# Expert stage of a fused attention and mixture-of-experts kernel: rows gathered in quarters and turned by VectorE, rows stored times their gate

## The reference, cut to what matters

```
logits = x @ w_gate
expert_idx = argmax(logits, axis=1)
probs = exp(logits - max) / (sum(exp(logits - max)) + 1e-9)
gate_w = probs[arange(N), expert_idx]
for e in range(E):
    xe = x[mask]                       # rows whose expert is e
    h = maximum(xe @ w1[e], 0.0)       # 512 -> 1024
    ye = h @ w2[e]                     # 1024 -> 512
    out[mask] = gate_w[mask, None] * ye
```

## Time and profile before

| | us |
|---|---|
| median of 3 runs (lowest, highest) | 1504.67 (1502.96, 1509.15) |
| the profiled execution: its time | 1505.98 |
| the profiled execution: span from first to last instruction | 1504.3 |
| PE busy in the span | 1470.9 |
| mean granted TensorE clock | 0.994 |

### The profile page before, as it was taken

How to read it: one execution, slowest core, us unless ns; L and a number is a source line. 1 busy time by engine, 2 the same in 40 slices (tenths; PEclk the granted TensorE clock), 3 DMA queues, 4 the chain that set the end, 5 groups by cost and what they waited for, 6 DMA issues and landing times.

```text
span 1504.3 us, 29653 instructions
## 1 busy us (share of the span) xinstructions
PE 1470.9 (98%) x8062; PEld 1273.0 (85%) x8063; DVE 882.0 (59%) x1629; ACT 619.4 (41%) x1295; POOL 524.2 (35%) x653
## 2 busy tenths in 40 slices
PE   7999999999989999999999999999999999999996
PEld 6999999999978888888888888888788878888885
DVE  5688888888835474755647375536455545553332
ACT  5688788778812222121222212133344334442221
POOL 5676676676710021120202112021333333332321
PEclk9999999999999999999999999999999999999998
DMA  6353443444430202021120202144767666643441
GB/s 249 120 141 102 105 112 101 110 106 119 112 129 0 67 18 84 0 84 27 57 65 19 84 0 84 27 133 137 254 234 222 225 203 235 229 167 133 139 142 40
DMA packets 111242, 173.49 MB, mean 115 GB/s; under 512 B 52976, under 2 KB 72176, under 8 KB 106978
## 3 DMA queue, kind: packets, MB, share of 16 engines
q1 hardware_dynamic: 103618, 152.82, 32.9%
q0 software_dynamic: 7584, 20.17, 4.2%
HBM read 123.66 MB, written 50.34 MB: 116 GB/s over the span
## 4 chain that ended last, share of the span: by engine, by line
PE 60%; DMA 5%; issue 3%; SPq 2%; ACT 1%; DVE 1%; ACTq 0%; POOL 0%; DVEq 0%; POOLq 0%
PE bank L167 58%; DMA arena<-we 3%; SPq L824 1%; DMA arena<-h_scratch 1%; ACT arena L1252 1%; PE bank L1710 1%; DMA h_scratch<-arena 1%; SPq L1013 0%; SPq L1005 0%; SPq L990 0%; PE bank L1641 0%; DVE hturn L1484 0%; ACT big L810 0%; PE bank L1649 0%; PE bank L1660 0%
## 5 line engine op out<-in xcount | busy, mean ns | idle before, releaser
L167 PE MATMUL bank<-big,xs 128*128 (+1 forms) x2100 | 495.4, 395 | 15.5 <-DVE big L610 8.1
L167 PEld LDWEIGHTS bank<-big,xs 128*128 128x128 f32 x2100 | 394.1, 190 | 98.1 <-issue 15.9
L167 PE MATMUL bank<-xs,big 128*128 128x512 f32 x1728 | 397.2, 391 | 2.7 <-PEq L216 2.7
L167 PEld LDWEIGHTS bank<-xs,big 128*128 128x128 f32 x1728 | 324.6, 188 | 70.2 <-issue 3.0
L167 PE MATMUL bank<-big 128*128 128x512 f32 (+1 forms) x1632 | 324.6, 347 | 2.0 <-POOL big L306 1.4
L167 PEld LDWEIGHTS bank<-big 128*128 128x128 f32 (+1 forms) x1632 | 254.7, 164 | 36.2 <-POOL big L306 1.7
L1045 POOL TENSOR_TENSOR arena<-arena 128x512 f32<-128x512 f32 x32 | 39.9, 1257 | 438.9 <-DMA arena<-rec_scratch 438.9
L1427 DVE TENSOR_TENSOR arena<-arena,bank 128x512 f32<-128x512 f32 x72 | 49.5, 687 | 242.4 <-PE bank L167 242.4
L1352 DVE CUSTOM_DVE_ANT_0 arena<-arena 128x512 f32<-128x512 f32 x256 | 159.6, 689 | 15.9 <-ACT arena L1204 14.8
L1184 ACT COPY arena<-bank 128x512 f32<-128x512 f32 x72 | 42.4, 589 | 305.5 <-PE bank L167 301.1
L704 PE MATMUL bank<-arena 128*128 128x66 f32 (+1 forms) x1152 | 147.7, 269 | 0.0
(11 more groups left out here) (182 smaller groups left out, 1360.7 us busy)
## 6 DMA issues: line engine op xcount, KB each, us to landing
arena<-we SPq DMA_DIRECT2D x32, 1024.0 KB, 7.7
h_scratch<-arena SPq DMA_DIRECT2D x37, 512.0 KB
arena<-h_scratch SPq DMA_DIRECT2D x148, 128.0 KB
kqraw<-kq SPq DMA_DIRECT2D x32, 576.0 KB, 3.8
rows_scratch<-arena SPq DMA_DIRECT2D x36, 256.5 KB
xT_scratch<-arena SPq DMA_DIRECT2D x32, 288.0 KB
arena<-v SPq DMA_DIRECT2D x64, 128.0 KB, 2.4
arena<-xT_scratch SPq DMA_DIRECT2D x8, 1024.0 KB, 5.5
```

The costliest lines, as they stand in the source:

```text
L167: ins = nc.tensor.matmul(out, left[a], right[b], start=first and n == 0, stop=last and n == 2)
```

## The change

Before the experts, the gate is no longer the 513th number of a row: ACT multiplies the four tiles of `x2` by it in place (`gated`), and SP stores 512 numbers a row. The relus have no scale, and the copies of gates between engines are gone.

In the loop, TensorE's transposes of the gathered rows are gone. POOL gathers a tile in four indirect DMAs (`gather_quarters`): block b of columns of `xg` gets, on each quarter of 32 partitions, a quarter (128 numbers) of the rows whose place in the tile lies in quarter b. DVE turns the 32x32 blocks (`turn_rows`, STREAM_TRANSPOSE 128x512 into `xturn`), ACT and DVE split that into high and low part as before, now from SBUF. The lists of row numbers for the quarters (`idq`) are laid out once by 16 DMAs that SP issues between the stages. The columns of `w_out` and the rows of `w_gate` are permuted on the host to fit. Tiles 0 to 3 are still gathered whole and turned by TensorE.

SP's step is reordered: `store_rows(g)`, then `load_quarters(g)`, then `loads_of(g - 1)`.

```diff
@@ SP, stage2
-                    sp.wait_ge(x2_sb, BQ * i + q + 1)
-                    if q == 0:
-                        sp.wait_ge(gates_done, i + 1)
+                    sp.wait_ge(x2_gated, BQ * i + q + 1)
                     sp.dma_start(m["rows"][ds(i * BT + q * P, P), :], x2[:, q]).then_inc(rows_out, 16)
...
             def tile(g):
-                load_quarters(g - 1)
                 store_rows(g, hs)
+                load_quarters(g)
                 loads_of(g - 1)
...
             for c in range(CPE, CPE + 3):
                 load(c)
+            sp.wait_ge(idf_set, 1)
+            idq = m["idq"][:].bitcast(U32).rearrange("p (b n) -> p b n", b=NQ)
+            for a in range(NQ):
+                for b in range(NQ):
+                    sp.dma_start(idq[a * Q:(a + 1) * Q, b], m["idf"][b * Q:(b + 1) * Q, :]).then_inc(idq_in, 16)
             sp.wait_ge(w_lo, CPE)
             sp.wait_ge(idt_mm, 1)
             sp.wait_ge(tabs, 2)
+            store_rows(2, hq)
+            load_quarters(2)
             load(CPE + 3)
-            store_rows(2, hq)
@@ POOL
+            def gather_quarters(g):
+                row = table(m, pool, ROW, g, 0, E * TPE - 1)
+                if isinstance(g, int):
+                    pool.wait_ge(xtr_mm, g)
+                else:
+                    pool.wait_ge(x_turned, g)
+                pool.sem_inc(turn_taken, 1)
+                pool.tensor_tensor(m["idgq"][:], idq[:, :, ds(row, 1)].rearrange("p b n -> p (b n)"),
+                                   m["quarter"][:, 0:1].to_broadcast([P, NQ]), ALU.add).then_inc(idg_set, 1)
+                pool.wait_ge(idg_set, g + 1)
+                pool.sem_inc(turn_taken, 1)
+                for b in range(NQ):
+                    pool.indirect_dma_start(xg[:, b * P:(b + 1) * P], None,
+                                            m["rows"].rearrange("r (a n) -> (r a) n", a=NQ),
+                                            bass.IndirectOffsetOnAxis(m["idgq"][:, b:b + 1], 0)).then_inc(xq_in, 16)
...
             gather(FIRST)
-            gather(FIRST + 1)
+            pool.wait_ge(idq_in, 16 * NQ * NQ)
+            gather_quarters(FIRST + 1)
...
             def period(g):
-                gather(g + 2)
+                gather_quarters(g + 2)
                 scatter(g - 2)
@@ ACT
+            def gated(i):
+                act.wait_ge(gates_done, i + 1)
+                for q in range(BQ):
+                    act.mul(x2[:, q], x2[:, q], rq[:, 3, q:q + 1]).then_inc(x2_gated, 1)
+            def turned_rows_high(g):
+                act.wait_ge(x_turned, g + 1)
+                act.copy(m["xt"][:, 0], m["xturn"]).then_inc(xt_hi, 1)
...
                 relu_stored(g)
-                rows_high(g + 1, False)
-                next_gate(g + 1)
+                turned_rows_high(g + 1)
                 turned_h_high(g - 1)
@@ DVE
+            def turn_rows(g):
+                dve.wait_ge(xq_in, 16 * NQ * g - 16 * NQ * FIRST)
+                dve.wait_ge(h_mm, 2 * g)
+                dve.transpose(m["xturn"].rearrange("p (c b j) -> p c b j", c=DC, b=P // Q),
+                              xg.rearrange("p (b i c) -> p c b i", b=P // Q, c=DC)).then_inc(x_turned, 1)
...
             def tile(g):
-                rows_low(g + 1)
+                turn_rows(g + 1)
+                turned_rows_low(g + 1)
                 turn_h(g - 1)
@@ PE
                 for h in range(2):
                     first_product(g, h, *here)
-                x_transpose(g + 1)
                 second_product(g - 2, *before)
```

More of the change, by code:

```diff
@@ L52 @@
 BQ = BT // P
-XW = DM + 1
+XW = DM
 TPE = N // P
@@ L63 @@
 SLOTS = 4
+NQ = 4
 PARTS = ((0, 0), (0, 1), (1, 0))
@@ L109, in alloc @@
     over("hturn", [FF], xs_at + (DC * BT + DM) * 4)
+    over("xturn", [DM], xs_at + DC * BT * 4)
     over("filler", [XW], xs_at)
@@ L138, in alloc @@
     m["hq"] = arena[:, SLOTS * CW:SLOTS * CW + FF]
+    m["cden"] = m["idq"][:, 0:H * S // DK]
     m["gw"] = m["stage"][:, 0:GMAX * E]
+    m["gi"] = m["stage"][:, CW // 2:CW // 2 + GMAX * E]
+    m["idf"] = arena[:, SLOTS * CW + 2 * FF:SLOTS * CW + 2 * FF + E * TPE].bitcast(U32)
     at = CW - 2 * P
@@ L595, in _ @@
             dve.memset(v[0:D, :, MID + 1], 0.0).then_inc(masks_set, 1)
+            for a in range(NQ):
+                dve.memset(m["quarter"][a * (P // NQ):(a + 1) * (P // NQ), :], a)
             def w3_low(j):
@@ L846, in stage2 @@
         idg_set, ids_set, turn_taken = sem("s3_idg_set"), sem("s3_ids_set"), sem("s3_turn_taken")
-        gate_set, relu_done = sem("s3_gate_set"), [sem(f"s3_relu_done{h}") for h in range(2)]
-        h_turned, gate_saved = sem("s3_h_turned"), sem("s3_gate_saved")
+        relu_done = [sem(f"s3_relu_done{h}") for h in range(2)]
+        h_turned, x_turned = sem("s3_h_turned"), sem("s3_x_turned")
+        idf_set, idq_in, xq_in = sem("s3_idf_set"), sem("s3_idq_in"), sem("s3_xq_in")
+        x2_gated = sem("s2_x2_gated")
         h_stored, hq_in = sem("s3_h_stored"), sem("s3_hq_in")
@@ L1076, in ids_of, with gather @@
                 pool.tensor_copy(m["idg"][:], m["idall"][:, ds(row, 1)]).then_inc(idg_set, 1)
-            def gather_rows(g):
+            def gather(g):
+                pool.wait_ge(xtr_mm, g)
+                ids_of(g)
                 pool.wait_ge(idg_set, g + 1)
@@ L1140, in period @@
             def period(g):
-                gather(g + 2)
+                gather_quarters(g + 2)
                 scatter(g - 2)
             last = tiles(pool, period, 2)
-            keep_gate(last)
             scatter(last_of(pool, 3))
@@ L1186, in turn @@
                         high(i, j - 1)
+                    if j == 4 and has_before(i):
+                        gated(i - 1)
                 high(i, FC - 1)
@@ L1251, in relu_half @@
                     product = product.rearrange("p (a k i) -> p a k i", a=2, i=Q)
-                act.activation(out, product, ACT.Relu, scale=m["gate"][:, 0:1]).then_inc(relu_done[h], 1)
+                act.activation(out, product, ACT.Relu).then_inc(relu_done[h], 1)
                 if h == 1:
@@ L1708, in x_transpose @@
                 pe.wait_ge(gathered, 16 * g + 16)
+                by_chunk = xg.rearrange("p (n c) -> p c n", c=DC)
                 for c in range(DC):
-                    last = pe.transpose(xtr_ps[:, c * P:(c + 1) * P], xg[:, c * P:(c + 1) * P], m["ident"][:])
+                    last = pe.transpose(xtr_ps[:, c * P:(c + 1) * P], by_chunk[:, c], m["ident"][:])
                 last.then_inc(xtr_mm, 1)
```

72 lines of the change are left out of this document (27 added, 45 removed).

## The result

The changed kernel takes 1512.62 us (median of 7 runs, 1511.4 to 1513.94), the kernel before 1506.29 us in the same series (7 runs, 1502.96 to 1509.19). The ratio is 1.0041 with a 95% interval of 1.003 to 1.0053. That is 0.4% slower: measurable here, but under the 0.5% that the prediction set as its bound for "slower", and about half of the 0.9% forecast. The profiled execution of the changed kernel has a span of 1512.2 us against 1504.3 before, so 7.9 us are to be explained.

The account below looks back on a forecast made before the run. TensorE, busy in 98% of the span, bounds the kernel, and SP's new round the loaded steps: 3.3 + 14.4 - 4.7 = +13.0 us on a span of 1504.3, forecast 1517.5 us; range 1491 to 1531, the forecast's own 1512 to 1531.

Parts of the forecast that it names:

- the step that decides: SP's queue in loaded loop steps: waiting for its own store's landing makes a round of 12.3 us, against 11.0 for PE.
- 2.0 + 2.5: SP's round: four quarter loads 2.0 us, then table reads and address work 2.5 us, ahead of the weight load.
- 20 steps from tile 6 on, +14.4: Loop steps holding 20 of 24 weight loads: 245.6 us with SP's new round against 231.2 before.
- in between: Rival for SP's round in the loop: 11.6 us a round, total about the same, 1504 us; chance 0.20.
- 36 x 0.36: Four TensorE transposes removed in each of the loop's 36 steps, 0.36 us a step: 13.0 us saved.
- lie beside products of 5 us: nothing: Dense blocks: ACT's eight times four gate multiplications, 0.6 us each, cost nothing.
- The ninth delays the last stores of rows: End of the dense blocks: ACT's ninth set of gate multiplications makes the last row stores some 1.6 us later.
- Lists and tile 4: Between the stages: 16 list DMAs at 0.5 us each delay tile 4's first product by 7.2 us; +8.9 with the clock.
- the rival of POOL's round: Loop: gathers stuck behind weight loads make POOL's round the bound, 11.9 us, 1515 us, up to 1540; chance 0.12.
- What would show it: Trace signs: four-group L1710, SP waiting for store landings, PE waiting 1.3 us a step, 8 us gap before tile 4.
- the faster rival: SP's round fits at 11.2 us: -12.7 us, 1492 us; sign: SP waits for the turn, PE unbroken; chance 0.28.

Follow-up runs that it names:

- g_whole_rows: Of the change only rows stored times their gate, scaled one copy earlier; whole gathers, TensorE transposes, old SP order: 1502.11 us, 0.9981 to the kernel before.
- b_new_sp: The kernel before with only SP's step in the changed order (store, its own quarters, weight load): 1504.71 us, ratio 0.9995.
- g_old_sp: The changed kernel with the gate scaling one copy earlier and SP's step in the old order: 1494.69 us, 0.9937 to the kernel before.

## Why the prediction was right or wrong, point by point

**The total.** The forecast was +13.0 us of span, measured +7.9; 1512.62 us lies in the range and at the edge of the forecast's own range (1512 to 1531). The sign was right, but that is luck in good part: two errors of 10 and 14 us, of opposite signs, nearly cancelled, so the total proves little. (By its own sum the forecast is 1504.67 + 13.0 = 1517.7 us and not 1517.5, which changes nothing.)

**SP's reordering, "the step that decides".** Mechanism right for the first half of the loaded steps: SP waits for its store's landing instead of for relus, the next quarters go out 7.56 us behind the weight load (foreseen 7.6 + 0.2), and undoing the order gives 10 to 12 us. Size wrong: the term "2.0 + 2.5" between quarters and weight load measured 3.94 us, of which the quarter loads are 1.92, so the table reads and address work take 2.0 us. The 2.5 us had been read between a store and a weight load, another place in the queue. The round is 11.50 and not 12.3 us. The failed step of the sum is "20 steps from tile 6 on, +14.4": it is +0.3 (ledger). 19 x 0.8 = 15.2 us for the shorter round cover the whole difference of 14. The prediction had written that a tenth in the round is 1.9 us; in effect its rival "in between" (a round of 11.6) describes the loop that ran.

**Transposes.** 36 x 0.36 was too small: a step without them is 10.88 us, not 11.0, so each step had spent 11.36 - 10.88 = 0.48 us on them, 17 us in all. The time from a group's start to the next matmul (0.35) left out the rest: the 48 matmuls up to the next group take 1140.99 - 1129.99 = 11.00 us, and without groups 10.88. Over the last 12 steps 5.3 us came back, where 4.7 were foreseen for 13.

**The transition.** The step that failed outright is "lie beside products of 5 us: nothing" together with "The ninth delays the last stores of rows". All nine sets of multiplications delay stores, and the eighth puts the last-but-one block's stores among the id scatters. The loss is 9.8 us there, by the start of tile 0's transposes, before and after:

```profile
1008.54 0.60 PE L1710 MATMUL bank<-ident,arena 128*128 128x128 f32 x4
```

```profile
1018.29 0.64 PE L1738 MATMUL bank<-ident,arena 128*128 128x128 f32 x4
```

1.9 of these were there before the gap's cause, the rest is the gap and the slow clock behind it. Both experiments that change the order of the two transfers take 0.4 to 0.5% back. The prediction asked whether ACT had time for the work and not what goes out later because of it.

**Lists and tile 4.** Foreseen +7.2 us for tile 4's start; measured 1079.67 - 1062.40 - 9.8 = 7.5. That is close only because errors cancel again: an issue took 10.62 / 16 = 0.66 us and not 0.5, over the upper bound of 9 us for the sixteen, and the four gathers took 5.9 us from 1067.80 on, the first of them 2.16 beside VectorE's work; but the copies began 4.8 us sooner than foreseen (1052.57 against 1047.6 + 9.8), since the third weight load was out sooner. That in turn is because the last rows land 4.2 us behind their first store's issue, here and in g_whole_rows, where the rows of 513 numbers took 9.2 us (8.2 in b_new_sp); the prediction had taken the 9.2 over. At tile 6 the loss without the transition is 13.9 - 9.8 = 4.1, foreseen 3.3.

**VectorE's turn.** Taken at 0.7, measured 1.08, between the bounds and near the upper. PE waited for L1483 for 3.3 us in all beside the first wait of 5.6.

**POOL.** Four gathers at 0.97 and 0.30 between them: measured 0.95 in the median (up to 2.16) and 0.30. Its round was put at 10.3 us, under 11.0, and that failed in the second half of the loaded steps: there it is on the chain that ended last, and from one tile's first gather to the next's takes 10.97, 11.31 and 11.05 us (1266.85, 1277.82, 1289.13, 1300.18), at or over the 10.88 that TensorE needs. The turn took 1.08 and not 0.7, and the landing came 2.5 to 3.0 us behind the last issue's end and not 2.4. So the rival of POOL's round, given 0.12, was in part true. Also not foreseen was that the scatter now goes out behind four gathers, so that VectorE's copy of the next result waits for its landing, in VectorE's waits from 1064 to 1490 us:

```profile
DVE arena L1490 <- DMA out<-arena,ids: 18.7, 8, 2.8
```

PE does not show it as a wait of its own. With the same gathers g_old_sp has no such wait of VectorE and runs at 11.0 us a loaded step, so it is a cost of the two together and not of the gathers alone.

**What would show it.** L1710's counterpart in four groups only: right. SP's waits: right for the landing; but SP also waits for the turn of the hidden rows, 67.8 us, which with an unbroken TensorE would have been the sign of the faster rival. PE waiting 1.3 us a step for `turned_h_low` (L1514): wrong, 2.6 us over 6 waits in all. The gap of some 8 us before tile 4's first product: 5.59.

## What to carry to other kernels

When work is put ahead of a store, cost the store's new place in time and not only the engine's: list what else is in flight then, above all scatters of tiny elements. A queue that waits for its own store's landing has a round of its own, and it costs little until the step becomes shorter than it; so a reorder that measures as neutral in one kernel can eat the gain of the next edit. And before small lists are moved by many DMAs on a queue that others need, see whether a matmul that copies partitions can do it: here 2.1 us of TensorE, 1.3 of ScalarE and 1.0 of GpSimd replaced 10.6 us of a queue.

## What was not expected of the hardware

- Four scatters of 128 4-byte ids each, issued within 5 us, were in flight with four row stores of 128x512 f32: the stores land 10.3 to 16.9 us behind their issue, and the DMA engines are busy 0.71 of the time at 10 GB/s. Apart from each other the stores are down by 982.3, 4.3 us behind the first issue. Issued ahead of most of the ids, the stores are waited for 9.5 to 9.9 us with the DMA engines nearly idle. A weight load issued behind the stores on their queue, which is not the ids' queue, took 23 us.
- VectorE's 32x32 transposes of 128x512 f32 with a source step of four numbers take 1.08 us, those of 128x1024 with none 1.25 us: per number 1.7 times as long, of which a fixed cost of an instruction is not taken out.
- With transposes on TensorE that read their rows at a step of four numbers, as in g_whole_rows, the step is 11.41 us and not 11.36. No run changes that alone.
